# Attention and routed expert layers in one kernel: the next batch's first scores ahead of the value products

## The reference

```python
# attention: q, k, v of shape (4, 8, 576, 64); a bias from relative positions through a small network
scores = scale * q @ k.T + bias
attn = exp(scores - max) / (sum + 1e-9)
x = (attn @ v) as 2304 rows of 512
# experts: P from x @ w_gate by 8 rounds of row and column normalisation
out = sum over 8 experts e of P[:, e] * (relu(x @ w1[e]) @ w2[e])
```

## Time and profile before

| | |
|---|---|
| device time, median of 3 runs | 1827.13 us (1827.11 to 1827.38) |
| device time of the profiled execution | 1827.18 us |
| its span, first to last instruction | 1825.4 us |
| TensorE busy | 1815.2 us, 99% |
| VectorE, GpSimd, ScalarE busy | 1038.2, 1031.1, 812.4 us |
| DMA | 157.72 MB, mean 86 GB/s |

### The profile page before, as it was taken

The page is one execution under the profiler, slowest core; times in us unless marked ns, Lnnn a source line. Parts: engine busy times, 40 slices in busy tenths (PEclk is TensorE's granted clock), DMA queues, the critical chain, the costliest instruction groups (busy, mean ns, idle before and its releaser), DMA issues.

```text
span 1825.4 us, 27577 instructions
## 1 busy us (share of the span) xinstructions
PE 1815.2 (99%) x10158; PEld 1590.1 (87%) x10158; DVE 1038.2 (57%) x1752; ACT 812.4 (45%) x1400; POOL 1031.1 (56%) x731
## 2 busy tenths in 40 slices
PE   8999999999999999999999999999999999999999
PEld 4687788888999999999999999999999999999998
DVE  9877777677555455556545553555455545554553
ACT  9777778534333333343334333333333333333331
POOL 0232346767666666657675666666666666656661
PEclk9999999999999999999999999999999999999999
DMA  7675662121121111212211111111221212211110
GB/s 249 197 204 138 161 165 75 47 74 65 70 70 70 69 70 70 70 70 104 70 69 70 62 61 66 67 70 70 70 104 70 70 70 70 70 70 70 70 47 35
DMA packets 51039, 157.72 MB, mean 86 GB/s; under 512 B 14320, under 2 KB 22896, under 8 KB 36592
## 3 DMA queue, kind: packets, MB, share of 16 engines
q1 hardware_dynamic: 50784, 156.14, 26.7%
q10 hardware_dynamic: 144, 0.09, 0.0%
HBM read 140.88 MB, written 15.34 MB: 86 GB/s over the span
## 4 chain that ended last, share of the span: by engine, by line
PE 96%; DVE 0%; issue 0%; DVEq 0%
PE banks L761 14%; PE banks L762 14%; PE banks L760 14%; PE banks L728 13%; PE banks L732 13%; PE banks L730 13%; PE banks L654 5%; PE banks L618 4%; PE banks L602 2%; PE banks L603 2%; PE banks L572 0%; PE banks L623 0%; PE banks L669 0%; PE banks L573 0%; PE banks L778 0%; PE banks L574 0%
## 5 line engine op out<-in xcount | busy, mean ns | idle before, releaser
L1447 POOL TENSOR_TENSOR w_lo<-stage,w_hi 128x1024 fp32r<-128x1024 f32 (+1 forms) x288 | 647.5, 2263 | 512.2 <-ACT w_hi L962 506.7
L762 PE MATMUL banks<-w_hi,h_lo 128*128 128x512 f32 x1152 | 450.1, 391 | 0.0
L761 PE MATMUL banks<-w_lo,h_hi 128*128 128x512 f32 x1152 | 449.9, 391 | 0.0
L760 PE MATMUL banks<-w_hi,h_hi 128*128 128x512 f32 x1152 | 449.0, 390 | 0.0
L1320 DVE SCALAR_TENSOR_TENSOR h_lo<-corner,h_hi 128x384 fp32r<-128x384 f32 x384 | 408.2, 1090 | 0.0
L1224 DVE TENSOR_TENSOR u<-p_copy,banks 128x384 f32<-128x384 f32 x96 | 53.1, 553 | 490.8 <-PE banks L732 490.8
L1010 ACT ACTIVATE h_hi<-corner 128x384 fp32r<-128x384 f32 x384 | 196.6, 526 | 271.0 <-DVE corner L1314 267.9
L728 PE MATMUL banks<-x_hi,w_hi 128*128 128x384 f32 x896 | 300.9, 336 | 0.0
L732 PE MATMUL banks<-x_hi,w_lo 128*128 128x384 f32 x896 | 300.2, 335 | 0.0
L962 ACT ACTIVATE w_hi<-stage 128x1024 fp32r<-128x1024 f32 (+1 forms) x288 | 271.6, 974 | 9.0 <-POOL stage L1441 8.4
L999 ACT ACTIVATE p_copy<-banks 128x384 f32<-128x384 f32 x96 | 47.3, 492 | 490.9 <-PE banks L732 490.9
(11 more groups left out here) (153 smaller groups left out, 2485.7 us busy)
## 6 DMA issues: line engine op xcount, KB each, us to landing
stage<-in_expert_w SPq DMA_DIRECT2D x96, 1024.0 KB, 4.7
raw<-in_qk SPq DMA_DIRECT2D x32, 576.0 KB, 6.8
bias_scratch<-bias_out SPq DMA_DIRECT2D x36, 288.0 KB, 2.9
bias<-bias_scratch SPq DMA_DIRECT2D x16, 288.0 KB, 4.7
bias<-bias_scratch SPq DMA_DIRECT2D x16, 256.0 KB, 5.2
v_main<-in_v SPq DMA_DIRECT2D x16, 256.0 KB, 2.8
bias<-in_last SPq DMA_DIRECT2D x16, 256.0 KB, 2.8
out<-total SPq DMA_DIRECT2D x4, 768.0 KB, 4.0
```

What stands on the lines that cost most here:

```text
L760: pe.matmul(dst, h_hi[:, g % 2, f, tokens], hi[:, f], start=fp == 0 and f == 0, stop=False)
L761: pe.matmul(dst, h_hi[:, g % 2, f, tokens], lo[:, f], start=False, stop=False)
L762: mm = pe.matmul(dst, h_lo[:, g % 2, f, tokens], hi[:, f], start=False, stop=fp == FPAIRS - 1 and f == 1)
L1447: pool.tensor_tensor(lo, of, hi.bitcast(F32), ALU.subtract).then_inc(w_split, 1)
```

## The change

On TensorE the scores of a batch's tile 0 (from the third batch on, `scored_ahead`) are no longer at the head of their own step but in the step in front, between the turn of tile 3 and the first burst of value products of the batch in front. The last pair's steps are written out instead of being a turn of the loop. In the turn of tile 4 the `fold` product for the last keys goes first and not last, with its waits. In the turn of tile 0 the heads are turned in the order 1, 0 and not 0, 1. On ScalarE the copy of turned head 0 of tile 4 goes behind both exponentials of the new tile 0 (`COPY_BETWEEN` without 0). On VectorE the second piece of the scaling goes behind the reading of tile 4, and the copy of the first half of the heads behind both readings of the new tile 0.

```diff
--- before.py
+++ after.py
@@ -69,7 +69,7 @@
 PV_DONE = (1, 2)
 HEADS_AT = (5, 6)
 REST_FIRST = (2, 3)
-COPY_BETWEEN = (0, 2, 3)
+COPY_BETWEEN = (2, 3)
 TAIL = 6
 LAST_SPREAD = 3
 TOK = N // P
@@ -609,7 +609,12 @@
                 at, qc = hp * STEPS + s, s % QC
                 if not exists(hp, s - 1):
                     pe.wait_ge(bias_evac, BIAS_TILES)
-                for h in range(2):
+                if qc == KC:
+                    pe.wait_ge(exped, reading(hp, s, 0) + 1)
+                    pe.wait_ge(kept_t[2], at)
+                    pe.matmul(rest_bank[:, 0:REST], probs[:, s % 2, KC * P:LAST_KEYS], fold[:], start=True,
+                              stop=True).then_inc(turned[2], 1)
+                for h in (1, 0) if qc == 0 and exists(hp, s - 1) else (0, 1):
                     pe.wait_ge(exped, reading(hp, s, h) + 1)
                     if exists(hp, s - 1):
                         pe.wait_ge(kept_t[h], at)
@@ -617,13 +622,11 @@
                         begin = main(h) + i * P if qc < KC else (h * KC // 2 + i) * P
                         mm = pe.transpose(banks[:, 4 + h, i * P:i * P + P], probs[:, s % 2, begin:begin + P], ident[:])
                     mm.then_inc(turned[h], 1)
-                if exists(hp, s - 1):
-                    pe.wait_ge(kept_t[2], at)
                 if qc < KC:
-                    mm = pe.transpose(rest_bank[:, 0:P], probs[:, s % 2, KC * P:KC * P + BOTH], ident[:])
-                else:
-                    mm = pe.matmul(rest_bank[:, 0:REST], probs[:, s % 2, KC * P:LAST_KEYS], fold[:], start=True, stop=True)
-                mm.then_inc(turned[2], 1)
+                    if exists(hp, s - 1):
+                        pe.wait_ge(kept_t[2], at)
+                    pe.transpose(rest_bank[:, 0:P], probs[:, s % 2, KC * P:KC * P + BOTH],
+                                 ident[:]).then_inc(turned[2], 1)
 
             def values(hp, s, part):
 
@@ -671,8 +674,12 @@
                         mm = pe.matmul(inverse_bank[:, at:at + REST], wide, fold[:], start=True, stop=True)
                 mm.then_inc(spread, 1)
 
+            def scored_ahead(hp, s):
+
+                return s % QC == 0 and exists(hp, s - 2 * QC) and exists(hp, s)
+
             def step(hp, s):
-                if exists(hp, s):
+                if exists(hp, s) and not scored_ahead(hp, s):
                     scores(hp, s)
                 for piece in range(PIECES):
                     if (s - 8 - piece) % QC == 0 and exists(hp, s - 8 - piece):
@@ -680,15 +687,19 @@
                 for early in (True, False):
                     if not early and exists(hp, s - 1):
                         turn(hp, s - 1)
+                    if not early and scored_ahead(hp, s + 1):
+                        scores(hp, s + 1)
                     for part, (after, _, _, before_turn) in enumerate(PV_PARTS):
                         if (s - after) % QC == 0 and exists(hp, s - after) and early == before_turn:
                             values(hp, s - after, part)
 
             for s in range(STEPS):
                 step(0, s)
-            with pe.Fori(1, PAIRS) as hp:
+            with pe.Fori(1, PAIRS - 1) as hp:
                 for s in range(STEPS):
                     step(hp, s)
+            for s in range(STEPS):
+                step(PAIRS - 1, s)
             def product(g, k):
 
                 w, which, fresh = PRODUCTS[k]
@@ -1183,8 +1194,6 @@
                     if (s - 8 - piece) % QC == 0 and exists(hp, s - 8 - piece):
                         scale_heads(hp, s - 8 - piece, piece)
 
-                heads_due(0)
-                scale_due(1)
                 for h in range(2):
                     if exists(hp, s) and not (qc == KC and h == 1):
                         if s < QC and h == 0:
@@ -1203,8 +1212,10 @@
                         if qc == 2 and exists(hp, s - 2):
                             keep_turned(hp, s - 2, 2)
                         scale_due(0)
+                scale_due(1)
                 if last and s == STEPS - QC + 1:
                     split_factor(0, 0)
+                heads_due(0)
                 heads_due(1)
                 for part in (() if not exists(hp, s - 1) else (1,) if qc == 1 else (2, 1) if qc in REST_FIRST else (1, 2)):
                     keep_turned(hp, s - 1, part)
```

## The result

The changed kernel takes 1832.98 us (median of 8 runs, 1832.89 to 1833.12), the kernel before 1827.18 in the same comparison: ratio 1.0032, 95% interval 1.0021 to 1.0042. It is slower by 5.8 us, 0.3%. The forecast was 1831.6, that is +4.45, with a range that ends at 1833.0: the side and the mechanism are right, the size is 1.4 us short, and that the median still lies inside the range, by 0.02 us, is luck.

What follows compares the result with a forecast made beforehand. TensorE, busy 99% of the span, bounds the kernel in its own program order; 2.4 + 0.9 + 1.4 - 0.25 = +4.45 us on 1827.18 gives 1831.6 us, range 1824.5 to 1833.0.

Steps and rivals of the forecast that it cites:

- first cycle: Cycle from 75.35, scores not yet moved: ScalarE's later copy holds the second burst 0.5 us; next last turn +0.9 us.
- 12 steady cycles: Batches between last turns at 91.72 and 288.41: TensorE waits for GpSimd's split, 16.59 against 16.39 us each, +2.4 us.
- cycle of the weight split: Cycle from 288.41: GpSimd splits expert weights before the batch's split; next last turn after 17.79 against 16.37 us, +1.4.
- last batch: No scores moved there; scores of tile 1 and tile 3 gain 0.18 + 0.06, so -0.25 us.
- What replaces it: Moved tile 0 scores before the first burst wait for GpSimd's two subtractions; TensorE stands 0.49 us, batch +0.20.
- the chain between this turn and GpSimd's start: New tile 0's turn to ScalarE's copy 1.13, copy to second rounding 0.48, rounding to GpSimd 1.23 us.
- The second term: Last batch, scaling behind the reading of the last keys: taken as 0, with 0.8 us kept once for the range.
- the gain at the scores of tile 1: On TensorE between last turn and second burst: 0.18 us gained, the burst at 1.86 instead of 2.04.
- The 0.06 at the scores of tile 3: Late restart on TensorE, 0.35 against 0.29 us on a late reading, which VectorE's earlier copy was to advance: 0.06 gained.
- What is removed: Scores of tile 1 stall twice on VectorE's reading of tile 0's scores: 0.11 each plus 0.05 bare wait, together 0.27 us.
- rival A: At the wait before the moved scores: GpSimd in time, not slower, 16.07 us a batch, 1824.9 us; chance 0.15.
- Rival B: ScalarE's moved copy holds the second burst in every batch, +0.52 in 12 more, 1837.8 us; chance 0.05.

## Why the prediction was right in kind and wrong in size

| part | forecast | in the trace |
|---|---|---|
| first cycle | +0.9 | 17.42 - 16.37 = +1.05 |
| 12 steady cycles | +2.4 | 200.02 - 196.69 = +3.33 |
| cycle of the weight split | +1.4 | 17.78 - 16.37 = +1.41 |
| last batch | -0.25 | +0.02 |
| sum | +4.45 | +5.8 |

**What replaces it: right in kind.** The moved scores wait for `split_done`, GpSimd's chain closes a loop from last turn to last turn, and the swap of heads sits in it: forecast 0.40 us, and once undone 0.42 (5.66 to 5.24) in most cycles, 0.35 in the rest. The release took 0.05, scores and first burst 3.83, the new tile 0 was turned at 4.45 (4.44 forecast).

**The step that failed: the chain between this turn and GpSimd's start,** which I put at 1.13 + 0.48 + 1.23 = 2.84, all from one batch. It took 2.94. The cycle was forecast at 16.59 and measured at 16.67, and these 0.08 twelve times are 1 us of the 1.4 that are missing. Two different small things fill it. In pairs 1 and 2, which run in a loop, GpSimd starts 0.07 after the rounding, as in the batch that I read, but ScalarE's copy, now awaited, starts at 5.66 and not 5.57. In pairs 0 and 3 the copy is at 5.58 as forecast, but GpSimd follows the rounding by 0.17; so it did before (7.41 to 7.58 after the last turn at 75.35), had I read a second batch. I took VectorE's start behind a turn as the price of ScalarE's; in the looped batches it is not. The first cycle is short by 0.15 in the same way: 0.10 behind the rounding, and a second burst at 2.61 instead of 2.55.

**The second term: the last batch.** I took 0 for the scaling behind the reading of the last keys and kept more for the range. It costs 0.2: the scaling ends 1.18 us after the start of the turn of tile 3 (323.10) and ended 0.76 after it, and that turn and the burst behind it are 1.28 us apart (321.92 to 323.20) and were 1.08:

```profile
321.92 1.04 PE L623 MATMUL banks<-ident,probs 128*128 128x128 f32 x8
...
323.20 2.16 PE L657 MATMUL banks<-probs_t,v_main 128*64 128x288 f32 x16
```

```profile
321.87 0.82 DVE L1207 CUSTOM_DVE_ANT_0 probs<-banks,bias 128x640 f32<-128x640 f32 x1
...
322.62 0.48 DVE L1166 TENSOR_TENSOR x<-heads,banks 128x320 f32<-128x320 f32 x1
```

```profile
316.35 1.04 PE L618 MATMUL banks<-ident,probs 128*128 128x128 f32 x8
...
316.62 0.49 DVE L1155 TENSOR_TENSOR x<-heads,banks 128x320 f32<-128x320 f32 x1 [0.39 <-PE banks L671]
```

That eats the gain at the scores of tile 1. The 0.06 at the scores of tile 3 that I expected from the earlier copy did not come, in the changed kernel or with the swap alone.

**What is removed: right.** The second burst comes 1.86 us after the last turn, as forecast, and came at 2.04. That the cycle with GpSimd out of the way is shorter by 0.27, the very number of the stalls at the scores of tile 1, is chance: 0.17 of it is what is gained there, less what the turn behind a burst costs, and 0.10 is gained around the first burst. That burst started 1.08 us after the turn of tile 3; the moved scores follow this turn after 0.91 and take 0.07 more where they now stand. These cycles are 16.12, rival A's 16.07 with the 0.06 that did not come. Rival A's condition, GpSimd in time, was false for this kernel, and the experiments that make it true give its price. **Rival B** (the copy holds the second burst in every batch) was rightly set aside for the changed kernel and is exactly what its ScalarE part does alone, 0.52 a cycle. The Trainium skill (TensorEngine Tiling, Key Properties) says that a change of tiling mode drains the engine; that it then costs alike in either order was my inference, and no run here isolates it.

## What to carry to other kernels

When work is moved forward on the engine that bounds, list what it waits for and put for each the time it is ready beside the new time it is wanted, both counted from one event of the cycle: GpSimd's split was ready at 12.9 and wanted at 15.2, and came to be wanted at 12.3. If the late chain itself starts from the bounding engine, its lateness recurs in every cycle, and each hundredth in it counts that many times: read its links in more than one batch, and in both looped and written-out code. A small reordering such as two heads swapped can be free in one schedule and nearly the whole loss in another, so try each part alone and undo each part in the whole.

## What the runs showed of the hardware that I had not expected

An engine released by the same kind of event did not always start equally fast. ScalarE's awaited copy started 1.13 us after the turn began in the batches whose steps are written out and 1.21 in those that run in a loop; GpSimd followed the end of the rounding by 0.17 us in written-out batches and 0.07 in looped ones. The looped batch is the one shown above (turn at 230.54, copy at 231.75, rounding until 233.40, GpSimd at 233.48); in a written-out one the rounding ends at 99.97:

```profile
97.19 1.09 PE L623 MATMUL banks<-ident,probs 128*128 128x128 f32 x8
...
98.32 0.60 ACT L923 ACTIVATE probs_t<-banks 128x512 f32<-128x512 f32 x1 [0.26 <-PE banks L623]
98.81 1.16 ACT L880 ACTIVATE qk_hi<-raw 128x1152 fp32r<-128x1152 f32 x1
...
100.14 2.67 POOL L1433 TENSOR_TENSOR qk_hi<-raw,qk_hi 64x1152 fp32r<-64x1152 f32 x1 [11.29 <-ACT qk_hi L880]
```

The same two values for GpSimd stand in the kernel before and with the swap undone. What makes the difference was not tried.
